# Attention stepped over batches within a block, k and v kept in place, and the first expert's weights split on ScalarE and VectorE

## The reference, cut to what matters

```python
# q, k, v: 4 batches, 8 heads, 576 positions, 64 dims each, float32
scores = matmul(q, k.T) / 8, masked to 0 <= i - j < 64; attn = softmax(scores)
x = (attn @ v) as rows: 2304 tokens x 512
# mixture of experts, 8 experts, w1[e] 512x1024, w2[e] 1024x512
noisy = x @ w_gate + log1p(exp(x @ w_noise)) * noise          # per token, 8 logits
two best experts per token, weights from a softmax over the two
y = sum over the two of weight * (relu(x @ w1[e]) @ w2[e])
# dense layer, w_in 512x2048, w_out 2048x512
h = y @ w_in;  g = h where h >= 1, 0 where h <= -1, (h + 1)^2 / 4 between
out = g @ w_out
```

## Time and profile before

| | |
|---|---|
| median of 3 runs | 1152.0 us (1148.45 to 1155.65) |
| profiled execution, device time | 1153.66 us |
| its span in the profile | 1152.0 us |
| busy: PE, DVE, ACT, POOL | 1091.4, 368.9, 347.4, 332.6 us |
| HBM read, written | 135.90 MB, 33.82 MB |
| granted TensorE clock, mean | 0.963 |

### The profile page before, as it was taken

How to read it: one execution, slowest core, us unless ns; L and a number is a source line. 1 busy time by engine, 2 the same in 40 slices (tenths; PEclk the granted TensorE clock), 3 DMA queues, 4 the chain that set the end, 5 groups by cost and what they waited for, 6 DMA issues and landing times.

```text
span 1152.0 us, 20177 instructions
## 1 busy us (share of the span) xinstructions
PE 1091.4 (95%) x6737; PEld 935.6 (81%) x6738; DVE 368.9 (32%) x637; ACT 347.4 (30%) x812; POOL 332.6 (29%) x235
## 2 busy tenths in 40 slices
PE   7987945999999999999999999989999999999998
PEld 5876833788878888888888888789898898998997
DVE  5577665112111211212212212262341332422421
ACT  4443440212211221221221222243252352442431
POOL 3014142643376160615244340661101101101000
PEclk9887866999999999999999999999999999999999
DMA  9997883688967372837464540461102101011000
GB/s 243 265 242 211 257 274 116 212 263 263 330 217 252 133 249 109 273 109 242 141 217 147 213 169 19 129 192 55 47 9 55 45 10 55 19 35 55 0 19 19
DMA packets 89260, 170.12 MB, mean 148 GB/s; under 512 B 29392, under 2 KB 34000, under 8 KB 88208
## 3 DMA queue, kind: packets, MB, share of 16 engines
q0 software_dynamic: 32176, 104.61, 28.4%
q1 hardware_dynamic: 44960, 43.11, 13.0%
q10 hardware_dynamic: 12096, 22.03, 5.6%
HBM read 135.90 MB, written 33.82 MB: 147 GB/s over the span
## 4 chain that ended last, share of the span: by engine, by line
PE 77%; DMA 11%; issue 6%; POOL 3%; SPq 2%; DVE 1%; ACT 0%; POOLq 0%; DVEq 0%
PE bank L1086 6%; PE bank L1084 5%; PE bank L1022 5%; PE bank L1085 5%; PE bank L1024 5%; PE bank L1007 5%; PE bank L1023 5%; PE bank L1009 5%; PE bank L1008 5%; PE bank L1070 5%; PE bank L1069 5%; PE bank L1071 5%; DMA x_sorted<-gath 4%; DMA gath<-x_rows,token_of 3%; PE bank L894 3%
## 5 line engine op out<-in xcount | busy, mean ns | idle before, releaser
L365 POOL TENSOR_TENSOR Wl<-stage,Wh 128x2048 fp32r<-128x2048 f32 x40 | 184.2, 4606 | 78.0 <-DMA Wh<-w 57.5
L1069 PE MATMUL bank<-zT_h,Wh 128*128 128x256 f32 x576 | 159.4, 277 | 1.0 <-DVE zT_l L833 1.0
L1071 PE MATMUL bank<-zT_h,Wl 128*128 128x256 f32 x576 | 159.3, 277 | 0.0
L1070 PE MATMUL bank<-zT_l,Wh 128*128 128x256 f32 x576 | 159.3, 277 | 0.0
L799 DVE COPY y_out<-bank 128x512 f32<-128x512 f32 x43 | 29.7, 692 | 372.7 <-PE bank L1024 347.0
L1007 PE MATMUL bank<-Wh,xT_h 128*128 x344 | 141.0, 410 | 5.0 <-POOL Wl L365 2.4
L1009 PE MATMUL bank<-Wh,xT_l 128*128 x344 | 136.9, 398 | 0.0
L1022 PE MATMUL bank<-Wh,hT_h 128*128 x344 | 135.6, 394 | 0.1
L1008 PE MATMUL bank<-Wl,xT_h 128*128 x344 | 135.7, 394 | 0.0
L1024 PE MATMUL bank<-Wh,hT_l 128*128 x344 | 135.0, 392 | 0.0
L1023 PE MATMUL bank<-Wl,hT_h 128*128 x344 | 133.6, 388 | 0.0
(11 more groups left out here) (152 smaller groups left out, 1665.4 us busy)
## 6 DMA issues: line engine op xcount, KB each, us to landing
stage<-w POOLq DMA_DIRECT2D x32, 1024.0 KB, 5.7
Wh<-w POOLq DMA_DIRECT2D x32, 1024.0 KB, 10.6
x_sorted<-gath SPq DMA_DIRECT2D x43, 256.0 KB
y_sorted<-y_out ACTq DMA_DIRECT2D x43, 256.0 KB
x_in<-x_sorted ACTq DMA_DIRECT2D x41, 256.0 KB
v_win<-vW SPq DMA_DIRECT2D x36, 256.0 KB, 5.0
k_ch<-kT SPq DMA_DIRECT2D x12, 512.0 KB, 6.3
q_bd<-qT SPq DMA_DIRECT2D x24, 192.0 KB, 4.9
```

What stands on the lines that cost most here:

```text
L365: nc.gpsimd.tensor_tensor(Wl[:, s, cols], stage[:, c % 2], Wh[:, s, cols], ALU.subtract).then_inc(w_ready, 1)
L1069: nc.tensor.matmul(here, high, zT_h[:, k], start=(k == 0), stop=False)
L1070: nc.tensor.matmul(here, high, zT_l[:, k], start=False, stop=False)
L1071: mm = nc.tensor.matmul(here, low, zT_h[:, k], start=False, stop=(k == KD - 1))
```

## The change

- **Order.** Attention steps run over the four batches within a block (`s = 4 i + b`), all 36 written out. Rows of 64 keys go to a ring of four slots and rows of 64 values to a ring of two halves for each batch, so each is loaded once; even and odd blocks get masks of their own. Queries come as one row of blocks for all batches, two slots, loaded when the row two before is scored. ScalarE issues the first k and v; the noise comes in one contiguous transfer.
- **Logits.** Two steps (two batches of one block) form 128 tokens, whose logits are made together (128 columns of weights, at every second step) and stay in PSUM; the two kinds of copies to `lg` are gone, and VectorE's routing starts with two operations on PSUM in place of one.
- **First expert.** Its raw quarters are loaded as before, its high part is made by ScalarE in 16 pieces of 128x512 (`cast_piece`, at every second step from step 4) and its low part by VectorE (`low_piece`, from step 5). GpSimd computes nothing in attention and routing after its constants.
- **All other weights.** GpSimd makes the high part from `stage` (`tensor_copy`, 128x2048), then subtracts; the converting transfers are gone. Expert 1's first half is made before the seventh gather (`t == 6`), its second half before the thirteenth (`t == 12`).

```diff
@@ sync
+            def step(s):
+                i, b = s // B, s % B
+                if b == 1 and i + 2 < BLOCKS:
+                    sp.wait_ge(scored, B * (i + 1))
+                    load_q(i + 2)
+                    if i >= 1 and i + 3 < BLOCKS:
+                        load_k(i + 3)
+                if i >= 1 and i + 1 < BLOCKS:
+                    sp.wait_ge(pv_done, s + 1)
+                    load_v(b, i + 1)
+                if s % 2:
+                    sp.wait_ge(x_ready, s + 1)
+                    store_x(s // 2)
@@ gpsimd
-            def low_part(n, s, c):
-                pool.wait_ge(w_cast[c // 2], 32 * n + 32)
-                pool.wait_ge(staged[c % 2], 32 * n + 16 * (c // 2) + 16)
+            def parts(n, s, c):
+                hold(staged[c % 2], 32 * n + 16 * (c // 2) + 16)
                 cols = slice(STG * c, STG * c + STG)
+                nc.gpsimd.tensor_copy(Wh[:, s, cols], stage[:, c % 2]).then_inc(high_ready, 1)
+                pool.wait_ge(high_ready, 4 * n - 4 + c + 1)
                 nc.gpsimd.tensor_tensor(Wl[:, s, cols], stage[:, c % 2], Wh[:, s, cols],
                                         ALU.subtract).then_inc(w_ready, 1)
-            def load_first(m, n, s, pace=(None,) * 6):
-                for c in range(4):
...
-                    pool.dma_start(dst, src).then_inc(w_cast[c // 2], 16)
+            def first_parts(m, n, s):
                 for c in range(2):
-                    low_part(n, s, c)
+                    parts(n, s, c)
                     hold(w_ready, 4 * n + c + 1)
-                    load_raw(m, c + 2, pace[4 + c])
+                    load_raw(m, c + 2)
+            def last_parts(n, s):
                 for c in range(2, 4):
-                    low_part(n, s, c)
+                    parts(n, s, c)
                 hold(w_ready, 4 * n + 4)
...
-            fetch_first(0, [(scored, 1), (scored, 4)])
-            load_first(0, 0, 0, [(scored, k) for k in (7, 10, 14, 18, 22, 26)])
-            load_rest(0, 0)
-            fetch_first(1, [(scored, 29), (scored, 32)])
-            load_first(1, 1, 1, [(scored, 34)] + [(x_ready, G)] * 5)
+            fetch_first(0, [(scored, 3), (scored, 6)])
+            for c in range(2):
+                load_raw(0, c + 2, (w_ready, c + 1))
+            fetch_first(1, [(w_ready, 3), (w_ready, 4)])
...
             for t in range(TILES):
-                if t == 8:
-                    load_rest(1, 1)
+                if t == 6:
+                    first_parts(1, 1, 1)
+                if t == 12:
+                    last_parts(1, 1)
@@ scalar
+            def cast_piece(k):
+                c, cols = k // PIECES, slice(PC * (k % PIECES), PC * (k % PIECES) + PC)
+                act.wait_ge(staged[c % 2], 16 * (c // 2) + 16)
+                nc.scalar.activation(Wh[:, 0, PC * k:PC * k + PC], stage[:, c % 2, cols], ACT.Copy).then_inc(piece_cast, 1)
...
-                if (i - 5) % CH == CH - 1 and has(g, 7):
-                    act.wait_ge(logits_done, g - 4)
...
+                if s >= 4 and s % 2 == 0 and s < 4 + 8 * PIECES:
+                    cast_piece((s - 4) // 2)
@@ vector
+            def low_piece(k):
+                c, cols = k // PIECES, slice(PC * (k % PIECES), PC * (k % PIECES) + PC)
+                dve.wait_ge(piece_cast, k + 1)
+                inst = nc.vector.tensor_tensor(Wl[:, 0, PC * k:PC * k + PC], stage[:, c % 2, cols],
+                                               Wh[:, 0, PC * k:PC * k + PC], ALU.subtract)
+                if k % PIECES == PIECES - 1:
+                    inst.then_inc(w_ready, 1)
...
+                if s >= 5 and s % 2 and s < 5 + 8 * PIECES:
+                    low_piece((s - 5) // 2)
...
-            then(nc.vector.scalar_tensor_tensor(t_a[:], z, -1.0, z, ALU.mult, ALU.min))
+            then(nc.vector.tensor_scalar(noisy[:], z, 0.0, None, ALU.max))
+            then(nc.vector.scalar_tensor_tensor(t_a[:], noisy[:], -2.0, z, ALU.mult, ALU.add))
@@ tensor
+            def logits(t):
...
+                for m in range(KD):
+                    mm = nc.tensor.matmul(LG_ps[:, 2 * E * t:2 * E * t + 2 * E],
+                                          xT_blk[:, m % 2, m // 2].rearrange("p u q -> p (u q)"), w_gn[:, m],
+                                          start=(m == 0), stop=(m == KD - 1))
...
+            for s in range(G + 5):
+                if s < G:
+                    scores(s)
+                if 2 <= s < G + 2:
+                    transposed_probs(s - 2)
+                if 3 <= s < G + 3:
+                    values(s - 3)
+                if 4 <= s < G + 4:
+                    transposed_x(s - 4)
+                if s >= 6 and s % 2 == 0:
+                    logits((s - 6) // 2)
```

More of the change, by code:

```diff
@@ L237, in _, with load_q @@
         def _(sp):
-            def load_chunk(b, c):
+            def load_q(r):
                 for hi in range(2):
                     rows = slice(64 * hi, 64 * hi + 64)
[L241 to L245, removed]
@@ L271, in _ @@
+            for at in (slice(0, 1), slice(1, 2), slice(2, 4)):
+                for hi in range(2):
+                    rows = slice(64 * hi, 64 * hi + 64)
+                    sp.dma_start(q_bd[rows, 0, at, :, hi].rearrange("p b j q -> p (b j) q"),
+                                 qT[0, rows, at].rearrange("p b (j q) -> p (b j) q", j=J)
+                                 ).then_inc(row0_loaded[at.start], 16)
+            load_q(1)
+            load_k(2)
+            load_k(3)
             sp.dma_start(w_gn[:, :, 0:E], w_gate.rearrange("(a p) e -> p a e", p=P)).then_inc(gn_loaded, 16)
@@ L281, in _ @@
-            for i in range(BLOCKS):
-                step(B - 1, i, True)
+            sp.dma_start(nz[:].rearrange("p t e -> p (t e)"), noise).then_inc(nz_loaded, 16)
+            for s in range(G):
+                step(s)
             sp.wait_ge(const_ready, ALL_CONSTANTS)
@@ L541, in _ @@
-            for i in range(BLOCKS):
-                step(0, i)
-            with act.Fori(1, B) as b:
-                for i in range(BLOCKS):
-                    step(b, i)
-            for i in range(4):
-                step(B, i)
-            act.wait_ge(logits_kept, G // CH - 1)
-            nc.scalar.activation(lg[Q:P, 0:NT - CH], lg[0:Q, NT:G - CH], ACT.Copy).then_inc(route_act, 1)
-            step(B, 4)
+                if s >= 5 and s % 2:
+                    t = (s - 5) // 2
+                    act.wait_ge(xT_done, s - 3)
+                    if t:
+                        act.wait_ge(logits_done, t)
+                    nc.scalar.activation(xT_blk[:].rearrange("p a h u q -> p (a h u q)"), XT_ps[:],
+                                         ACT.Copy).then_inc(xT_copied, 1)
@@ L553, in _ @@
+            first_k(slice(2, 4))
+            for b in range(1, B):
+                first_v(b)
+            for s in range(G + 4):
+                step(s)
             act.wait_ge(route, ROUTE_NEGABS)
             nc.scalar.activation(sp_t[:], t_a[:], ACT.Exp).then_inc(route_act, 1)
-            act.wait_ge(route_act, 2)
+            act.wait_ge(route_act, 1)
             nc.scalar.activation(rest[:], sp_t[:], ACT.Ln, bias=1.0).then_inc(route_act, 1)
@@ L692, in _ @@
-            for i in range(3):
-                step(B, i)
+                        rowinv[:, k % 2].unsqueeze(2).to_broadcast([P, J, Q]), ALU.mult).then_inc(x_ready, 1)
+                if s >= 5 and s % 2 and s < 5 + 8 * PIECES:
+                    low_piece((s - 5) // 2)
+            for s in range(G + 3):
+                step(s)
             n = [0]
@@ L946, in _, with scores @@
-            for i in range(BLOCKS):
-                step(0, i)
-            with pe.Fori(1, B) as b:
-                for i in range(BLOCKS):
-                    step(b, i)
-            for i in range(5):
-                step(B, i)
+            keep_busy(banks[7], 12)
+            pe.wait_ge(const_ready, FIRST_CONSTANTS)
+            def scores(s):
+                i, b = s // B, s % B
+                if i == 0:
+                    pe.wait_ge(row0_loaded[min(b, 2)], 48)
+                elif b == 0:
+                    pe.wait_ge(q_loaded[i % 2], 32 * ((i + 1) // 2))
+                    if i >= 2:
+                        pe.wait_ge(k_loaded[i % 4], 16 * ((i + 2) // 4 if i % 4 >= 2 else i // 4))
+                if s in (0, B):
+                    pe.wait_ge(zeroed, 2 * i + 2)
+                if s in (B, 2 * B):
+                    pe.wait_ge(const_ready, ODD_CONSTANTS if i % 2 else EVEN_CONSTANTS)
+                if s >= 3:
+                    pe.wait_ge(exp_done, s - 2)
+                mask = mask_first if i == 0 else mask_odd if i % 2 else mask_even
+                nc.tensor.matmul(S_ps[s % CH][:].rearrange("p (j n) -> p j n", j=J), ident_b[:],
+                                 mask[:].unsqueeze(1).to_broadcast([P, J, P]), start=True, stop=True)
+                even, odd = (k_slot(max(i, 1) - (max(i, 1) + e) % 2) for e in range(2))
```

(25 more changed lines are left out.)

332 lines of the change are left out of this document (133 added, 199 removed).

## The result

The changed kernel takes 1141.2 us in the median (four runs, 1140.15 to 1142.83), beside 1153.7 us for the kernel before on the same chip (four runs, 1148.45 to 1155.65). The ratio is 0.990, 95% interval 0.985 to 0.994: about 1% faster where 2.8% was forecast, and inside the range. The profiled execution took 1140.15 us, its span is 1138.6 us: 13.4 under the span before.

A forecast was written before the change was run, and what follows sets the result against it. TensorE, busy 95% of the span, was taken as the bound, losing time in attention and routing. Terms -21.4 +1 -3 -4 -1.2 -8.7 +8 -2.5 = -31.8 gave 1121 us, range 1107 to 1145.

The forecast's parts named there:

- The step that failed: Behind attention and routing: TensorE's granted clock is near nine tenths and its work is unchanged, so no term for it.
- Subtractions: Attention: with GpSimd's subtractions gone, the stalls of VectorE's scalings and TensorE's steps vanish, -21.4 us.
- the stalls stay: Rival, attention and routing: scaling waits for something other than the subtraction; some 25 us stay, total 1146, chance 0.03.
- Loads of the start: First attention steps: the queue jam goes and k and v load once, -3 us, between 7.2 regained and 4 lost.
- logits: Attention: one group of logit matmuls for two steps, 0.89 us against 1.14, saves 0.125 a step, -4 us.
- Pieces on VectorE: Attention: sixteen pieces of the first expert's low part mostly fill VectorE's waits, cost 1 us, at most 12.
- the pieces and the first loads are exposed: Rival, attention: TensorE waits for VectorE every second step (+11) and for first loads and piece (+7), 1139, chance 0.13.
- Start of routing: Routing's beginning: the last copies of logits go, one operation of 0.31 us is added, -1.2 us.
- routing: Routing chain: two 128x144 operations of 4.15 and 5.19 us fall to 0.31 each, -8.7 us.
- the rivals in which GpSimd's copies are dear: Ahead of expert 2: copy at 6.3 us, total 1147, chance 0.09; or 9 us, 1163 and more, chance 0.05.
- a second one wins back four gathers' spacing (about 1.1 us each): -4: Gathers: a second GpSimd pause empties four buffers, recovering 4 us; last gather 16 us later, expert 2 +8.
- The last weights: Quarters of `w_out`: loads start without converting transfers, waits of 2.9 us shrink to about 0.4, -2.5 us.

The follow-up runs named there:

- moved version: Changed kernel with 32 unused bytes per partition ahead of each stage's tiles, so they start at multiples of 64 bytes: 1122.1 us.
- sixth experiment: Changed kernel with tiles moved back by 32 bytes, plus four unused GpSimd subtractions and one fill in attention: 1152.8 us.

## Why the prediction was right or wrong

Measured by spans: 43.3 us gained up to the first gather, 14.4 lost from there to expert 2, and 15.5 lost from there to the end, -13.4 in all. The forecast had -37.3, +8 and -2.5. That 1141.2 lies inside the range is luck: the range reached up to 1145 for exposed pieces and a dearer copy, and neither happened.

**The step that failed** is the sentence "Behind it TensorE is at nine tenths nearly everywhere, and the change leaves its work there alone". The instructions are the same; their operands' addresses are not. I read the diff for instructions and transfers and passed over a constant whose type changed. Moving the tiles back by 32 bytes gives 17.8 us of that stretch and 19.1 of the whole, and moving them in the kernel before costs 15.3. The sum had this term at nothing. The 17.8 come out of the counts: 32 tiles x 0.2 = 6.4, and eight steps from one dense group to the next x 1.40 = 11.2. The moved version is at 1122.1, beside the 1121 forecast; that is partly luck, since up to the first gather it gained 5.8 us more than forecast and from there to expert 2 it lost 5.6 us more.

**Up to the first gather** the terms were right or too small:
- Subtractions (-21.4): right. No step from 10 to 34 is stalled, so the rival "the stalls stay" falls. Put back, four subtractions cost 25.9 us in the new order.
- Loads of the start (-3) and logits (-4): too small together. Attention up to step 34 gained 34.5 us; without the 21.4 that is 13.1, where these terms and the pieces had 6. Step 10 came 6.6 us earlier; the first steps still wait for queries, 2.20 us in the row at 10.62. The step itself went from 3.20 to 2.93, 9.7 us in 36, where I had 4: one group of logits costs 0.80 for a pair instead of 0.57 for each, and the masking matmul takes 0.22 or 0.23 in the chain instead of 0.32. The two make up the whole 0.27, which leaves nothing for the loop written out, as forecast. Rows of the chain (start, duration, line, count):

```profile
86.38 0.80 PE bank L966 x8
87.18 0.23 PE bank L920
```

  In the sum 0.89 stood for the logits, the nearest row; it was 0.80.
- Pieces on VectorE: sixteen of 0.68 us, and the step got shorter all the same. The rival "the pieces and the first loads are exposed" falls.
- Start of routing (-1.2) and routing (-8.7): right to 1 us. From step 34's masking matmul to the first gather it takes 40.1 us instead of 48.9, and no operation of 128x144 is above 0.31.

**From the gathers to expert 2** the price of the copy was right (1.90), so the rivals in which GpSimd's copies are dear fall; 23.6 us behind the last gather were forecast as 22. Wrong was "a second one wins back four gathers' spacing (about 1.1 us each): -4". After the pause four gathers start 1.3 us apart, but the fifth waits 5.18 us for the sorted write of the first: what four empty buffers save, the write behind them takes back. Start to start the two pauses take 17.2 and 14.9 us, against 10.9 for the one before, and all other gathers are 2.3 us apart on average, against 2.2. From first to last it took 21.7 us longer, not 16, and TensorE lost 14.4 where I had 8.

**The last weights** (-2.5): right. The moved version shows it alone, 2.3 less than the kernel before from expert 2 to the end.

Why did 32 bytes move at all? In attention the new rings leave SBUF nearly full: the last tile ends at 229216 of 229344 bytes. The constant's old size would need 288 more; 32 more fit.

What stays open: why an operand 32 bytes past a multiple of 64 costs TensorE some 5 ns a matmul. The runs show that it does, for 256 and 512 columns alike, so it is a price for each matmul and not for each column. The fast starts above all lie 64 past a multiple of 128, the slow ones 32 or 96 past it; other offsets, a multiple of 128 among them, were not tried for these operands.

## What to carry to other kernels

Compare where the operands of the hot matmuls start as well as the instructions: one constant that changes size moves every tile allocated behind it. When time is missing in a stretch without waits and at full clock, compare the mean durations of the same line before and after. Here a shift by the same few nanoseconds everywhere came from the operands, and not from the order. A short piece of work that another engine needs at one point should not stand behind a long list on an in-order engine: expert 2's weights behind 43 gathers cost 20 us, and nothing among them.

## What the runs showed of the hardware

- Operands of TensorE in the reduced format that start 32 bytes past a multiple of 64: 281 instead of 276 ns for 256 columns streamed, and 12.36 to 12.37 instead of 12.17 us for a tile, in two kernels. The matmuls of attention read plain f32 operands, which were 32 bytes off in the changed kernel too. They took the same with and without (274 ns for 128 columns). The Trainium skill (SBUF — State Buffer, Operand start alignment) asks for a start at a multiple of the element size and says that this is "about legality, not speed"; all these starts keep it, so the speed is shown by the runs alone.
- A fill on GpSimd held VectorE as a subtraction does. In the sixth experiment's timeline:

```profile
24.04 3.85 DVE L708 TENSOR_SCALAR bias<-negmax 128x4 f32<-128x4 f32 x1
...
24.33 3.53 POOL L456 MEMSET Wl<- 128x4096 f32 x1
24.44 3.44 DVE L714 COPY probsT<-bank 128x512 f32<-128x512 f32 x1
```

  All three end together, at 27.9. The copy reads PSUM, not SBUF; it may have been held itself or by the scaling ahead of it, which the runs don't tell apart.
